# A tile's product within its chunk, issued one step sooner on TensorE

## The chip, the cores and the metric

The kernel runs on one core of a Trainium2 chip. The metric is the device time of one execution in microseconds (us). A time given for a kernel is the median over several executions.

## The reference

Three stages follow each other. The first is a recurrent attention (mLSTM) over 4 batches, 8 heads, 768 tokens and a head size of 40; the other two are dense layers over the 3072 tokens x 320 that it gives.

```python
for t in range(S):                                   # S = 768, for each batch and head
    m_new = np.maximum(f_gate[t] + m, i_gate[t])
    f_stab, i_stab = np.exp(f_gate[t] + m - m_new), np.exp(i_gate[t] - m_new)
    m = m_new
    C = f_stab * C + i_stab * outer(v[t], k[t])      # 40 x 40
    n = f_stab * n + i_stab * k[t]
    y[t] = sigmoid(o_gate[t]) * (C @ q[t]) / np.maximum(abs(n @ q[t]), 1.0)
x = relu(x @ w_in) ** 2 @ w_out                      # 3072x320, 320x2048, 2048x320
x = elu(x @ w_in2) @ w_out2
```

## The kernel before, in words

**Tiles.** The recurrence is computed by chunks of 128 tokens. A tile g is one chunk of one batch with its 8 heads, so there are 24 tiles: g = 4 * chunk + batch. Three tiles make a block, 8 blocks for each dense layer. A layer works through a block in 16 steps, one for each slice of 128 of the 2048 hidden columns. A step t (0 to 255, 0 to 127 for the first layer) issues on TensorE `first_product(t)`, 8 matmuls of 128x384 at L933 in float32r, and `second_product(t - 3)`, 9 matmuls of 128x320 at L947.

**What is between the two products.** The attention of tiles 3 to 23 is woven into the steps of the first layer. For tile g, `start_of(g)` is its first step s (1, 6 and 11 for tiles 3, 4 and 5; after that 16 * (g // 3 - 1) + 5 * (g % 3) - 1), and `tile_at(t, delay)` gives the tile whose s + delay is t. TensorE executes in the order in which it is written out by hand:

- step s: `scores(g)`, q times k for each head, L823, into the PSUM banks A0 and A1; it waits until tile g - 1 is finished (`den_ready`) and for the low part of q (`q_lo`)
- step s + 2: `state_added(g)`, 16 instructions at L838 (the chunk's own k and weighted v, into A2; for tile 3 it is in its step 3, and the last chunk has none), then `from_state(g)`, 6 instructions at L849 (q times the state of the chunks before, into A0; none for tile 3, which is of the first chunk)
- step s + 3: `within(g)`, 16 instructions at L858 (the weighted scores in `wts` times v, into A1)
- step s + 5: `x1_transposed(g)`, three transposes of the finished tile (L863 and L864)

These attention products are plain float32, which is two instructions for each.

**The other engines for tile g.** VectorE in step s multiplies the scores into `wts` (`weigh`, L629, two halves; each raises `p_ready`). `from_state` waits for the first half, `within` for both. In step s + 3 VectorE runs in this order: `update_state` (L640, L643), `add_inter` (L651), the low part of this step's activations (`glo`, L773, which needs ScalarE's L546, L549 and L550 behind `first_product(s + 3)`), in the first block the low parts of a later slice's weights (L688, L690), then `finish(g)`: L660 (waits for `within(g)` by `intra_ps`) to L673 (`den_ready`) and the copy L676 (`x_ready`). ScalarE splits the next tile's k (L443) and q (L448); GpSimd makes the low part of q (`split_q_lo`, L342, two halves), the mask (L347) and the weighted v (L359). A DMA queue (SP) loads the next tile's q and k (L258) when the low part of the present q is made, then k, v and o (L266) and the row of maxima (L247).

**Waits that bear on the moved call.**

```python
def within(g):
    kvo_loaded(pe, g)
    pe.wait_ge(s["p_ready"], 2 * g + 2)
```

Of the kernel before, what the change touches and what calls it, by code (L numbers as in the profile page):

```python
# [50 lines left out]
def start_of(g):  # L51

    if g < 2 * T:
        return (1, 6, 11)[g - T]
    return NF * (g // T - 1) + 5 * (g % T) - 1


def tile_at(t, delay):

    for g in range(T, TILES):  # L60
        if start_of(g) + delay == t:
            return g
    return None


def transposed_at(t):

    return 2 * T - 1 if t == NF - 1 else tile_at(t, 5) if t != NF else None


def mlstm_two_dense_layers(nc, gates_ends, gates_inner, qk, q_trios, kvo, w_all, m_dram, out):
    with ExitStack() as ctx:
# [734 lines left out]
        def _(pe):  # L807
            def scores(g):
                if g < B:
                    pe.wait_ge(s[f"qk_in_{g}"], 16)  # L810
                    q_h, k_h = q_raw(g), k_raw(g)
                else:
                    pe.wait_ge(s["k_lo"], with_state(g) + 1)
                    q_h, k_h = q3, k3
                if g >= T:
                    pe.wait_ge(s["den_ready"], g)
                if g == T:
                    pe.wait_ge(s["decay_ready"], 1)
                for u, bank in enumerate(score_banks(g)):
                    if g >= B:  # L820
                        pe.wait_ge(s["q_lo"], 2 * with_state(g) + u + 1)
                    for h in range(HH):
                        last = nc.tensor.matmul(bank[:, h * P:(h + 1) * P], k_h[:, u * HH + h, :], q_h[:, u * HH + h, :],  # L823
                                                start=True, stop=True)
                    last.then_inc(s["s_ps"], 1)

            def state_added(g):
                if chunk_of(g) == CH - 1:
                    return
                pe.wait_ge(s["wv_ready"], g + 1)  # L830
                if g == 0:
                    pe.wait_ge(s["a_col_ready"], 2)
                elif g <= T:
                    pe.wait_ge(s["state_ready"], g)
                else:
                    pe.wait_ge(s["xt_ready"], g)
                for h in range(H):
                    last = nc.tensor.matmul(A2[0:D, h * E:(h + 1) * E], k_of(g)[:, h, :], wv[:, h, :], start=True, stop=True)  # L838
                last.then_inc(s["dc_ps"], 1)

            def from_state(g):
                if chunk_of(g) == 0:
                    return
                pe.wait_ge(s["state_in"], 48 * (with_state(g) + 1))
                pe.wait_ge(s["trio_in"], 16 * (with_state(g) + 1))
                pe.wait_ge(s["p_ready"], 2 * g + 1)
                for i in range(TRIOS):
                    n = min(3, H - 3 * i)
                    last = nc.tensor.matmul(A0[:, 3 * i * EV:(3 * i + n) * EV], q_of_three[0:n * D, i, :],  # L849
                                            state_diag[0:n * D, i, 0:n * EV], start=True, stop=True)  # L850
                last.then_inc(s["inter_ps"], 1)
# [4 lines that stand above are left out]
                bank = score_banks(g)[1]  # L856
                for h in range(H):
                    last = nc.tensor.matmul(bank[:, h * E:(h + 1) * E], wts[g % 3][:, h, :], v_of(g)[:, h, :], start=True, stop=True)  # L858
                last.then_inc(s["intra_ps"], 1)
# [6 lines left out]
            def x1_transposed(g):  # L866
                pe.wait_ge(s["x_ready"], g + 1)
                if g == 0:
                    pe.wait_ge(s["p_ready"], 1)
                elif g < T:  # L870
                    pe.wait_ge(s["xt_ready"], g)
                else:
                    pe.wait_ge(s["state_ready"], to_state(g + 1))
                transposed(x1[g % 2], x1[g % 2][:, 2 * P:3 * P], x_bank(g))

            def x2_transposed(i, w):
                pe.wait_ge(s["acc_free"], i + 1)
                pe.wait_ge(s["rest_ready"], i + 1)
                pe.wait_ge(s["xt_ready"], TILES + i - T + 1)
                if i < T:  # L880
                    pe.wait_ge(s["den_ready"], TILES)
                transposed(x2[:, i, :], x2_rest[i % 2][:].rearrange("p a n -> p (a n)"), (A0, A1, A2)[w])
# [40 lines left out]
            def first_product(t):  # L923
                block, j = divmod(t, NF)
                if j == 0:
                    pe.wait_ge(s["xt_ready"], T * (block + 1))
                if block % BLOCKS == 0:
                    win_lo_done(pe, NF * (block // BLOCKS) + j)
                wait(pe, "relu_ready" if block < BLOCKS else "g_ready", t - 1)
                hi, lo = xth[block % 2], xtl[block % 2]  # L930
                parts = [(0, hi, 0), (3, hi, 0), (0, lo, 0), (1, hi, 1), (4, hi, 1), (1, lo, 1), (2, hi, 2), (2, lo, 2)]
                for i, (w, x, kk) in enumerate(parts):
                    last = nc.tensor.matmul(hps[t % 2][:, 0:NT], win[:, j, w, :], x[:, kk, :], start=(i == 0),  # L933
                                            stop=(i == len(parts) - 1))
                last.then_inc(s["h_ps"], 1)

            def second_product(t):
                block, j = divmod(t, NF)
                pe.wait_ge(s["glo_ready"], t + 1)
                if block % BLOCKS == 0:  # L940
                    pe.wait_ge(s["wout_lo"], NF * (block // BLOCKS) + j + 1)
                for u in range(T):
                    if j == 0:
                        wait(pe, "acc_free", T * block + u - T + 1)
                    cols = slice(u * P, (u + 1) * P)
                    for i, (g, w) in enumerate(((ghi, 0), (ghi, 1), (glo, 0))):
                        last = nc.tensor.matmul(acc[u][:, 0:DM], g[t % GR][:, cols], wout[:, j, w, :],  # L947
                                                start=(j == 0 and i == 0), stop=(j == NF - 1 and i == 2))
                    if j == NF - 1:
                        last.then_inc(s["g_used"], 1)  # L950
                if j < NF - 1:
                    last.then_inc(s["g_used"], T)

            for block in range(2 * BLOCKS):
                for j in range(NF):
                    t = NF * block + j
                    if j == 0 and block > 0:
                        second_product(t - LAG)
                    first_product(t)
                    if t in FIRST_STATES:  # L960
                        state_added(FIRST_STATES[t])
                    g = transposed_at(t)
                    if g is not None and g >= 2 * T:
                        x1_transposed(g)
                    g = tile_at(t, 0)
                    if g is not None:
                        scores(g)
                    g = tile_at(t, 2)
                    if g is not None:
                        if g > T:  # L970
                            state_added(g)
                        from_state(g)
                    g = tile_at(t, 3)
                    if g is not None:
                        within(g)
                    if BLOCKS - 1 <= block < 2 * BLOCKS - 1 and j in X2_STEPS:
                        w = X2_STEPS.index(j)
                        x2_transposed(T * (block + 1 - BLOCKS) + w, w)
                    if t >= LAG and j > 0:
                        second_product(t - LAG)  # L980
                    g = transposed_at(t)
                    if g is not None and g < 2 * T:
                        x1_transposed(g)
# [47 lines left out]
```

## Time and profile before

| | |
|---|---|
| median of 3 runs | 843.82 us (843.19 to 845.56) |
| the profiled execution's own time | 845.63 us |
| its span, first to last instruction | 843.5 us |
| granted TensorE clock, mean over the span | 0.982 |
| steps with attention on TensorE | 46 to 440 us, roughly |

The profiled execution took 845.63 us, of which 843.5 are its span and 2.1 lie around it. It was 1.8 us above the median of the runs. Positions below are microseconds from the start of the span. A row of the order of time names start, duration, engine (PE is TensorE's matmul, PEld its weight load, DVE VectorE, ACT ScalarE, POOL GpSimd), line, operation and operands; several neighbours of one kind are one row with their count (x16), and the brackets give idle time before the row and what ended it.

### The profile page before, as it was taken

The numbers are of one execution on the slowest core, as the hardware profiler recorded it, in microseconds if no ns is written. First come the engines' busy times: TensorE is split into PE (matmuls) and PEld (weight loads), VectorE is DVE, ScalarE is ACT, GpSimd is POOL, SyncE is SP. The second block draws the span as 40 slices with busy tenths as digits, with TensorE's granted clock in tenths as the row PEclk, the third lists the DMA queues.
The fourth block names the chain that finished last, engine by engine and source line by source line (L and its number), as shares of the span: only waits on it lengthen the run. The fifth ranks groups of instructions, "written<-read, shape, count | busy, mean of one in ns | idle before, by whom it ended". The sixth has DMA issues, their size and how long they took to land.

```text
span 843.5 us, 14970 instructions
## 1 busy us (share of the span) xinstructions
PE 833.7 (99%) x5568; PEld 821.9 (97%) x5568; DVE 467.3 (55%) x823; ACT 492.0 (58%) x1088; POOL 263.9 (31%) x291
## 2 busy tenths in 40 slices
PE   8999999999999999999999999999999999999998
PEld 7899999999999999999999999999999999999998
DVE  4798776665665766656636644443434444444442
ACT  4698676776766767677658754444444444444443
POOL 2654221322222222211102353333433333333332
PEclk7599999999999999999999999999999999999999
DMA  8685444453643443445132300000000000000000
GB/s 240 244 236 142 128 117 108 108 138 86 162 138 95 121 118 108 108 107 152 38 103 70 103 1 2 24 1 24 1 24 1 24 1 24 1 24 1 1 24 24
DMA packets 28256, 66.93 MB, mean 79 GB/s; under 512 B 9400, under 2 KB 15384, under 8 KB 25624
## 3 DMA queue, kind: packets, MB, share of 16 engines
q1 hardware_dynamic: 27608, 64.54, 27.1%
q10 hardware_dynamic: 576, 1.44, 0.5%
q8 instruction: 44, 0.72, 0.4%
q14 instruction: 28, 0.23, 0.1%
HBM read 60.87 MB, written 4.03 MB: 77 GB/s over the span
## 4 chain that ended last, share of the span: by engine, by line
PE 96%; DMA 2%; DVE 1%; POOL 0%; issue 0%; ACT 0%; SPq 0%; DVEq 0%
PE hps L933 42%; PE acc L947 40%; PE att L858 5%; PE att L823 2%; PE att L849 2%; PE att L838 2%; PE att L863 1%; DMA raw<-in_qk 1%; PE att L864 1%; DVE gate L618 0%; PE acc L823 0%; DMA x<-in_gates_ends 0%; DMA m_rows<-x 0%; DVE x L673 0%; POOL wout L384 0%
## 5 line engine op out<-in xcount | busy, mean ns | idle before, releaser
L933 PE MATMUL hps<-xth,win 128*128 128x384 f32 x1280 | 350.7, 339 | 0.0
L947 PE MATMUL acc<-wout,ghi 128*128 128x320 f32 x1536 | 347.5, 313 | 0.0
L933 PE MATMUL hps<-xtl,win 128*128 128x384 f32 x768 | 260.0, 339 | 0.0
L947 PEld LDWEIGHTS acc<-wout,ghi 128*128 128x128 f32 x1536 | 257.8, 188 | 0.0
L947 PE MATMUL acc<-wout,glo 128*128 128x320 f32 x768 | 237.7, 309 | 0.0
L933 PEld LDWEIGHTS hps<-xth,win 128*128 128x128 f32 x1280 | 229.5, 188 | 0.3
L431 POOL TENSOR_TENSOR glo<-hact,ghi 128x384 fp32r<-128x384 f32 x128 | 130.1, 1016 | 217.2 <-ACT ghi L593 217.2
L773 DVE TENSOR_TENSOR glo<-hact,ghi 128x384 fp32r<-128x384 f32 x128 | 80.2, 627 | 144.7 <-ACT hact L550 143.2
L933 PEld LDWEIGHTS hps<-xtl,win 128*128 128x128 f32 x768 | 144.9, 189 | 0.0
L947 PEld LDWEIGHTS acc<-wout,glo 128*128 128x128 f32 x768 | 144.1, 188 | 0.0
L588 ACT ACTIVATE hact<-hact 128x384 f32<-128x384 f32 x128 | 67.2, 525 | 130.4 <-DVE hact L795 130.4
L546 ACT ACTIVATE hact<-hps 128x384 f32<-128x384 f32 x128 | 62.5, 488 | 118.2 <-PE hps L933 117.0
L795 DVE TENSOR_SCALAR hact<-hps 128x384 f32<-128x384 f32 x128 | 71.2, 556 | 104.6 <-PE hps L933 104.6
L798 DVE SCALAR_TENSOR_TENSOR hact<-hact,hps 128x384 f32<-128x384 f32 x128 | 71.0, 555 | 76.6 <-ACT hact L588 76.6
L593 ACT ACTIVATE ghi<-hact 128x384 fp32r<-128x384 f32 x128 | 67.3, 526 | 74.5 <-DVE hact L798 74.5
L347 POOL TENSOR_SCALAR_AFFINE_SELECT wts<-wts 128x1024 f32<-128x1024 f32 x24 | 26.2, 1092 | 189.6 <-ACT wts L469 189.6
L342 POOL TENSOR_TENSOR q<-raw,q 40x512 fp32r<-40x512 f32 x40 | 51.9, 1315 | 84.7 <-ACT q L448 84.6
L549 ACT ACTIVATE ghi<-hact 128x384 fp32r<-128x384 f32 x128 | 67.2, 525 | 4.1
L550 ACT ACTIVATE hact<-hact 128x384 f32<-128x384 f32 x128 | 65.0, 508 | 0.0
L469 ACT ACTIVATE wts<-wts,a_col 128x128 f32<-128x128 f32 x192 | 60.4, 387 | 5.5 <-DMA wts<-m_rows 5.5
L618 DVE RECIPROCAL gate<-gate 128x320 f32<-128x320 f32 x24 | 51.5, 2145 | 0.1
L858 PEld LDWEIGHTS att<-kvo,wts 128*128 128x128 f32 x336 | 42.0, 198 | 0.2 <-issue 0.2
(136 smaller groups left out, 664.5 us busy)
## 6 DMA issues: line engine op xcount, KB each, us to landing
raw<-in_qk SPq DMA_DIRECT2D x20, 960.0 KB, 7.2
wts<-m_rows SPq DMA_DIRECT2D x24, 512.0 KB, 8.7
kvo<-in_kvo SPq DMA_DIRECT2D x21, 484.0 KB, 7.9
x<-in_w_all SPq DMA_DIRECT2D x12, 352.0 KB, 7.0
wts<-in_w_all SPq DMA_DIRECT2D x12, 352.0 KB, 3.0
q_of_three<-in_q_trios SPq DMA_DIRECT2D x20, 180.0 KB, 2.6
out_x<-hsum SPq DMA_DIRECT2D x16, 160.0 KB, 1.9
x<-in_w_all ACTq DMA_DIRECT2D x4, 352.0 KB, 6.7
```

The source lines that it names most:

```text
L431: nc.gpsimd.tensor_tensor(glo[t % GR][:], gfull[t % 2], f32(ghi[t % GR][:]), ALU.subtract)\
L546: nc.scalar.activation(relu[t % 2], hps[t % 2][:, 0:NT], ACT.Relu).then_inc(s["relu_ready"], 1)
L549: nc.scalar.activation(ghi[t % GR][:], relu[t % 2], ACT.Square).then_inc(s["ghi_ready"], 1)
L550: nc.scalar.activation(gfull[t % 2], relu[t % 2], ACT.Square).then_inc(s["g_ready"], 1)
L588: nc.scalar.activation(relu[t % 2], relu[t % 2], ACT.Exp).then_inc(s["e_ready"], 1)
L593: nc.scalar.activation(ghi[t % GR][:], gfull[t % 2], ACT.Copy).then_inc(s["ghi_ready"], 1)
L773: nc.vector.tensor_tensor(glo[t % GR][:], gfull[t % 2], f32(ghi[t % GR][:]), ALU.subtract)\
L795: nc.vector.tensor_scalar(relu[t % 2], hps[t % 2][:, 0:NT], 0.0, None, ALU.min).then_inc(s["hneg_ready"], 1)
L798: nc.vector.scalar_tensor_tensor(out=gfull[t % 2], in0=relu[t % 2], scalar=-1.0, in1=hps[t % 2][:, 0:NT], op0=ALU.add, op1=ALU.max).then_i ...
L858: last = nc.tensor.matmul(bank[:, h * E:(h + 1) * E], wts[g % 3][:, h, :], v_of(g)[:, h, :], start=True, stop=True)
L933: last = nc.tensor.matmul(hps[t % 2][:, 0:NT], win[:, j, w, :], x[:, kk, :], start=(i == 0), stop=(i == len(parts) - 1))
L947: last = nc.tensor.matmul(acc[u][:, 0:DM], g[t % GR][:, cols], wout[:, j, w, :], start=(j == 0 and i == 0), stop=(j == NF - 1 and i == 2))
```

## The change

`within(g)` is no longer called in step s + 3 but in step s + 2, directly behind `from_state(g)` and ahead of that step's `second_product`. For tile 3 that is behind `state_added(3)` in step 3. Nothing is added or left out, and no other engine's order is changed.

```diff
@@ -970,8 +970,6 @@
                         if g > T:
                             state_added(g)
                         from_state(g)
-                    g = tile_at(t, 3)
-                    if g is not None:
                         within(g)
                     if BLOCKS - 1 <= block < 2 * BLOCKS - 1 and j in X2_STEPS:
                         w = X2_STEPS.index(j)
```

## Rows read from the trace of the kernel before

**Rows 1.** Busy time by stretch: us, then each engine's busy time and count, clock, DMA.

```profile
46.00:98.00 52.00, 50.43 (x371) 48.52 (x371) 45.70 (x75) 42.07 (x98) 21.63 (x20) 1.00 0.69 190
98.00:440.00 342.00, 342.00 (x2455) 337.25 (x2455) 210.94 (x355) 235.52 (x526) 71.45 (x64) 1.00 0.42 112
```

**Rows 2.** Waits of TensorE's weight loads, 48 to 100 us: total, times, longest.

```profile
PEld att L823 <- issue: 2.4, 3, 1.3
```

**Rows 3.** Order of time, TensorE's matmuls around tile 15.

```profile
273.80 0.90 PE L849 MATMUL att<-state_diag,q_of_three 120*128 120x126 f32 x6
...
274.87 0.31 PE L947 MATMUL acc<-wout,glo 128*128 128x320 f32 x1
...
277.13 0.34 PE L933 MATMUL hps<-xtl,win 128*128 128x384 f32 x1
...
279.38 0.31 PE L947 MATMUL acc<-wout,glo 128*128 128x320 f32 x1
...
281.64 0.33 PE L933 MATMUL hps<-xtl,win 128*128 128x384 f32 x1
...
282.10 0.31 PE L947 MATMUL acc<-wout,glo 128*128 128x320 f32 x1
```

**Rows 4.** Order of time in three narrow stretches, weight loads around tile 15.

```profile
273.55 0.20 PEld L838 LDWEIGHTS att<-wv,kvo 128*40 128x40 f32 x3
...
274.01 0.53 PEld L849 LDWEIGHTS att<-state_diag,q_of_three 120*128 120x128 f32 x4
274.46 0.30 PEld L947 LDWEIGHTS acc<-wout,ghi 128*128 128x128 f32 x2
...
278.53 0.53 PEld L858 LDWEIGHTS att<-kvo,wts 128*128 128x128 f32 x4
278.98 0.30 PEld L947 LDWEIGHTS acc<-wout,ghi 128*128 128x128 f32 x2
```

**Rows 5.** Order of time, VectorE and TensorE, tile 21.

```profile
382.72 1.28 DVE L629 TENSOR_TENSOR wts<-wts,att 128x512 f32<-128x512 f32 x2
...
386.89 0.79 PE L849 MATMUL att<-state_diag,q_of_three 120*128 120x126 f32 x6
```

**Rows 6.** Order of time, tile 3 (VectorE, TensorE, ScalarE).

```profile
46.87 1.29 DVE L629 TENSOR_TENSOR wts<-wts,att 128x512 f32<-128x512 f32 x2
...
46.97 0.81 PE L838 MATMUL att<-wv,x 128*40 128x41 f32 x16
...
50.54 1.87 PE L858 MATMUL att<-x,wts 128*128 128x41 f32 x16
...
52.48 0.47 ACT L546 ACTIVATE hact<-hps 128x384 f32<-128x384 f32 x1
...
54.41 0.56 DVE L773 TENSOR_TENSOR glo<-hact,ghi 128x384 fp32r<-128x384 f32 x1
...
58.36 0.49 DVE L673 TENSOR_TENSOR x<-att,rden 128x320 f32<-128x320 f32 x1
```

**Rows 7.** Order of time, tile 4, GpSimd.

```profile
73.49 3.22 POOL L342 TENSOR_TENSOR q<-raw,q 40x512 fp32r<-40x512 f32 x2
```

**Rows 8.** Order of time, tile 5, ScalarE and VectorE.

```profile
88.90 0.49 ACT L546 ACTIVATE hact<-hps 128x384 f32<-128x384 f32 x1 [1.75 <-PE hps L933]
...
89.85 0.51 ACT L550 ACTIVATE hact<-hact 128x384 f32<-128x384 f32 x1
...
91.27 0.54 DVE L773 TENSOR_TENSOR glo<-hact,ghi 128x384 fp32r<-128x384 f32 x1
...
93.17 0.49 DVE L673 TENSOR_TENSOR x<-att,rden 128x320 f32<-128x320 f32 x1
```

**Rows 9.** Order of time, tile 7, GpSimd, VectorE and TensorE.

```profile
125.91 2.53 POOL L342 TENSOR_TENSOR q<-raw,q 40x512 fp32r<-40x512 f32 x2 [4.84 <-ACT q L448]
...
127.35 1.14 DVE L676 COPY x<-x 128x64 f32<-128x64 f32 x1
...
130.47 0.38 PE L863 MATMUL att<-ident,x 128*128 128x128 f32 x2
```

## What the change will do to the time

> **What bounds the kernel now.** I read the busy times by stretch first. Behind 98 us TensorE is busy without a gap through all steps that carry attention; in the first block, 46 to 98 us, it is idle for 1.6 us, and there VectorE is busy 45.7 of 52 us [rows 1]. So TensorE sets the time, and VectorE is next to it in the first block alone. The view of waits says where those gaps are: three times the weight loads of `scores` (L823) wait, 2.4 us in all [rows 2]. Their places follow from the order of time. `scores(4)` begins when VectorE ends `finish(3)` at 58.36 + 0.49 = 58.85 us [rows 6], `scores(6)` when it ends `finish(5)` at 93.17 + 0.49 = 93.66 us [rows 8], `scores(5)` likewise at 77.6 us. The clock is at its full level, 2.4 GHz, in both stretches [rows 1]. A TensorE instruction that vanished, a gap that the move puts into TensorE, and a `finish` that comes later in the first block all go straight into the time. Everything else is covered.
>
> **What a group costs where it is now.** From the last L933 ahead of `within(15)` to the first `glo` matmul of L947 behind it is 279.38 - 277.13 = 2.25 us; in the step after, without attention, the same stretch is 282.10 - 281.64 = 0.46 us [rows 3]. So `within` costs 1.79 us. Its 16 instructions are paced by their weight loads: four take 278.98 - 278.53 = 0.45 us, 0.112 each, hence 16 x 0.112 = 1.79 us [rows 4].
>
> **What it costs behind `from_state`.** The loads of L849 go at the same pace, four in 274.46 - 274.01 = 0.45 us, and the load of another group follows the last at that pace, with no pause [rows 4]. The way out is the same too: from the first L947 load to the `glo` matmul is 274.87 - 274.46 = 0.41 us behind L849 and 279.38 - 278.98 = 0.40 us behind L858 [rows 3, 4]. So 16 loads put in between cost 16 x 0.112 = 1.79 us, what they cost where they were. One exit from float32 to float32r goes, which costs about 0.09 us (0.38 us from the first L947 matmul to the `glo` one against 0.28 us without attention ahead); but the group also had an entry behind L933 where its first load ran under a long matmul, and that cover goes with it. The term is 0.00 us for each of 20 tiles. The transition L849 to L858 is not in the trace, so I keep bounds. Below: the exit's 0.09 us is won and the lost cover costs nothing, -1.7 us over 20 tiles. Above: the nearest dear transition is from L838 to L849, where three loads at 0.04 each take until 273.80 - 273.55 = 0.25 us, 0.13 us of it a pause [rows 3, 4]; 20 x 0.13 = +2.6 us. I take 0, since L849 into L947 is the nearer row: equally wide weights on both sides, and no pause.
>
> The Trainium skill, TensorEngine Tiling (Array Packing), Key Properties, says that changing the tiling mode drains TensorE. Trace and rule agree at L838 to L849 (40 columns to 128) [rows 3, 4]; whether 80 rows to 128 is such a change no row shows. Were it one, it would be the upper bound above.
>
> **Does the moved call wait?** It needs both halves of `weigh` instead of one. The second ends least early in tile 21, at 382.72 + 1.28 = 384.00 us, 2.9 us before L849 begins [rows 5]; of tiles 4 to 23 none is nearer. Its v is part of the load that `state_added` and the gates have used already. Tile 3 is the exception: VectorE begins `weigh` at 46.87 us and ends it at 48.16 us, while TensorE is through with L838 at about 46.97 + 0.73 = 47.70 us [rows 6]. TensorE will stand for some 0.5 us, with `second_product(0)` and step 4 queued behind. What follows: `first_product(4)`, over at 50.7 us, just behind the start of L858 [rows 6], ends 0.5 + 1.79 = 2.3 us later, at 53.0. ScalarE took it up at 52.48 us anyway, now at about 53.05; VectorE's L773 at 54.41 us [rows 6] would begin some 0.15 us later, and so would `finish(3)`, for which `scores(4)` already waits 1.3 us [rows 2]. The 0.5 us stall is thus swallowed by that wait: **+0.15 us** for tile 3. Without the wait in `scores(4)` it would be +0.5.
>
> **The other engines see step s + 3 late.** `within` now stands ahead of `second_product` of s + 2, so `first_product(s + 3)` ends 1.79 us later, although TensorE as a whole is level again one product later. ScalarE's L546 follows it at once, and through L550 the L773 of VectorE that stands ahead of `finish(g)`.
>
> Tile 5 pays for it in full. ScalarE had waited 1.75 us for the product, so L546 would begin at 88.90 + 1.79 = 90.69 us and L550 end at 89.85 + 0.51 + 1.79 = 92.15; L773 begins just behind, at 92.18 instead of 91.27 us: `finish(5)` is 0.9 us late, and `scores(6)` waits for its L673 already [rows 2, 8]. No `intra_ps` wait gives it back, since VectorE was not waiting for one. **+0.9 us**.
>
> Tile 4: VectorE is late enough by itself that L773 moves by only 0.1 us. But the split of q moves by 1.79 us: GpSimd's pair of L342 would begin at about 75.3 instead of 73.49 us, and takes 2.6 to 3.2 us [rows 7], until 77.9 to 78.5 us. The second half of `scores(5)` needs it at 78.05 us, so it waits 0 to 0.45 us. On the other side the weights' low parts then escape the overlap with L342 (-0.3). I take **+0.1 us**.
>
> Tiles 6 to 23: TensorE stands nowhere from there on [rows 1], and a move of 1.79 us counts only where less than that is in hand. `scores` stands behind the transposes and needs L673 and the end of L342, in tile 7 at 127.3 and 128.44 us, over 2 us ahead of it [rows 9]. The transposes are closer. In tile 7 the copy L676 takes 1.14 us and ends at 128.49 us, with GpSimd's L342 (125.91 + 2.53 = 128.44), though it copies only 64 columns [rows 9]. Both move by 1.79 us: to 130.28 us. The transposes' weights load 0.17 us ahead of 130.47 us [rows 9], at 130.30. With the 0.07 us that a released load needs (58.85 to 58.92) this is 0.05 us late, partly under the last L933. It is so for the tiles of the first two places in a block, 12 in all (in the third, q is split a step later); 12 x 0.02 = **+0.25 us**.
>
> The Trainium skill, SBUF — State Buffer, SBUF: two separate sides, has GpSimd and some VectorE operations lock one pair of ports for a whole instruction. Rows 9 agree. Without such a lock the copy would be over before L342, and the 0.25 would be 0.
>
> Sum: 0.00 + 0.15 + 0.9 + 0.1 + 0.25 = +1.4 us. Against the profiled execution, 845.6 + 1.4 = 847.0 us; against the median, which lies 1.8 us lower, 843.8 + 1.4 = **845.2 us**, 0.17% more. A measurement of this kernel tells about 0.3% (2.5 us) from nothing, so my forecast is no change.
>
> **The rivals.**
> 1. The saved exit is real: TensorE wins 0.09 us in each of 20 tiles, 1.7 us, against 1.4 us lost: 843.5 us. For it speaks the 0.38 against 0.28 us; against it that the group is paced by loads. Chance 0.14.
> 2. The transition L849 to L858 pauses, as L838 to L849: +2.6 + 1.4 = 4.0 us, 847.8 us. It decides from 0.06 us for a tile on. Against it stands L849 to L947. Chance 0.08.
> 3. The transposes become late in the 12 tiles: if `x_ready` comes 0.15 to 0.3 us behind the point at which they are due (0.05 by my sum, and GpSimd's start is the uncertain part), 12 x 0.2 = 2.4 us comes in place of 0.25: 847.4 us. From 0.12 us for a tile on it is slower by over 0.3%. Chance 0.11.
> 4. Faster beyond doubt: the exit is won and the first block loses nothing, because its waits (2.4 us) shrink with the group gone from step s + 3: -1.7 - 1.5 = -3.2 us, 840.6 us. Against it, those waits are for `finish`, which waits for L773 and not for `within`. Chance 0.04.
>
> My own sum keeps 0.63, range 844.0 to 846.6 us.
>
> **How the numbers follow.** The predicted time is the sum's. Range 843.0 to 848.0 us: it holds the sum's case, most of rival 1 and about two thirds of rivals 2 and 3. Faster by over 0.3% (under 841.3): rival 4, 0.04. Slower (over 846.35): half of rivals 2 and 3 and a tenth of my own case, as the size in the first block is uncertain, 0.17. Within: 0.79.
>
> **What the changed profile would show.** L858's loads directly behind L849's at 0.112 us, with 1.79 us from one to the next group's load; a wait of 0.4 to 0.5 us before L858 in tile 3; a shorter wait at the first L823 of the three, a longer one (about 1.5 instead of 0.66 us) at the third; L676 still ending with L342 and the transposes without a wait over 0.1 us. The prediction is wrong if L858 pauses behind L849, if the transposes or `scores` wait behind 98 us, or if the granted clock leaves its upper level there.

## The result: slower by 0.57%, outside the range

The changed kernel takes 848.70 us (median of 6, 848.02 to 850.40) against 843.51 us for the one before (median of 6, 842.83 to 845.56): ratio 1.0057, interval 1.0040 to 1.0074. The prediction was 845.2 us, 843.0 to 848.0, and 0.79 for no change. In a second measurement of both kernels (below, 6 and 29 executions) the ratio was 1.0044, interval 1.0030 to 1.0058.

The profiled execution took 848.02 us with a span of 845.9, which is 2.4 us above the profiled one of before, and it took 0.7 us less than the median of its kernel, while that of before lay 2.1 us above its own (845.63 against 843.51). So one trace against the other shows only half of the difference of the medians. The rest had to be looked for in more traces.

**What came as predicted.** The product within the chunk stands directly behind `from_state`. In the order of time of the changed kernel, tile 15 (TensorE's matmuls):

```profile
275.08 0.90 PE L849 MATMUL att<-state_diag,q_of_three 120*128 120x126 f32 x6
...
277.94 0.31 PE L947 MATMUL acc<-wout,glo 128*128 128x320 f32 x1
```

From the first L849 to the first `glo` matmul are 2.86 us, against 274.87 - 273.80 = 1.07 us before [rows 3]: the group costs 1.79 us here, to the hundredth what it cost in its old place. The transition has no price. In tile 3 TensorE waits for the second half of `weigh`, as expected, though for 0.25 us in this trace (0.5 in E2's) where 0.4 to 0.5 was foreseen (order of time, 47 to 50 us):

```profile
48.26 1.95 PE L858 MATMUL att<-x,wts 128*128 128x41 f32 x16 [0.25 <-DVE wts L629]
```

**What waits now.** The view of waits of the changed kernel, weight loads, first 48 to 100 us, then 100 to 440 us (total, times, longest):

```profile
PEld att L823 <- issue: 1.9, 2, 1.6
...
PEld att L823 <- POOL q L342: 0.2, 1, 0.2
```

```profile
PEld att L838 <- issue: 3.5, 14, 0.3
PEld acc L947 <- issue: 2.8, 6, 0.5
```

The L838 row was there before as well and is no wait for data. The L947 row is new: six waits of 0.47 us of the weight load each, and in the one worked out below the matmul comes 0.35 us late. Busy times by stretch, to lay beside [rows 1], show TensorE no longer without a gap behind 98 us:

```profile
46.00:98.00 52.00, 50.39 (x372) 48.60 (x370) 43.48 (x75) 42.08 (x98) 21.23 (x20) 1.00 0.65 179
98.00:440.00 342.00, 340.92 (x2442) 334.34 (x2442) 219.46 (x355) 233.48 (x524) 73.51 (x64) 1.00 0.42 114
```

One of the six, step s + 3 of tile 15, in the order of time of the changed kernel (ScalarE and the weight loads):

```profile
280.54 0.49 ACT L546 ACTIVATE hact<-hps 128x384 f32<-128x384 f32 x1 [2.56 <-PE hps L933]
...
281.91 1.04 ACT L448 ACTIVATE q<-raw 120x1024 fp32r<-120x1024 f32 x1
282.86 1.06 ACT L501 ACTIVATE x<-acc 128x320 f32<-128x320 f32 x3
...
283.38 0.30 PEld L947 LDWEIGHTS acc<-wout,ghi 128*128 128x128 f32 x2 [0.47 <-issue]
```

and the same work of ScalarE in the kernel before:

```profile
278.87 1.04 ACT L448 ACTIVATE q<-raw 120x1024 fp32r<-120x1024 f32 x1
279.82 1.22 ACT L501 ACTIVATE x<-acc 128x320 f32<-128x320 f32 x3
```

L501 empties the three accumulator banks at the end of a block. It stands in the block's step 2, which for the first tile of each block is just s + 3, and behind L448 in ScalarE's order. ScalarE waited 2.56 us for the late product, and everything behind it moved with it: L501 from 279.82 to 282.86 us, of which 1.28 us is that this trace is later as a whole by then (the first L849 of tile 15 at 275.08 against 273.80 us) and 1.76 us is the move. The next step's `second_product` starts a new accumulation in these banks, and was due one L933 behind 282.90, at 283.07 us; it began at 283.42 (PE), when the first copy was done. Six times 0.35 us are 2.1 us.

**Tile 5.** Order of time of the kernel before, weight loads:

```profile
93.73 0.97 PEld L823 LDWEIGHTS att<-q,k 120*128 120x128 f32 x8 [0.66 <-issue]
```

and of the changed kernel, VectorE and weight loads:

```profile
91.48 0.56 DVE L773 TENSOR_TENSOR glo<-hact,ghi 128x384 fp32r<-128x384 f32 x1 [1.46 <-ACT hact L550]
...
93.39 0.49 DVE L673 TENSOR_TENSOR x<-att,rden 128x320 f32<-128x320 f32 x1
...
93.95 0.97 PEld L823 LDWEIGHTS att<-q,k 120*128 120x128 f32 x8 [1.59 <-issue]
```

VectorE now waits 1.46 us for the product ahead of L773, and `scores(6)` waits 1.59 us instead of 0.66: 0.9 us more, as worked out. TensorE came to it 0.7 us sooner (93.95 - 1.59 = 92.36 against 93.73 - 0.66 = 93.07 us), thanks to tiles 3 and 4, so `scores(6)` starts only 0.2 us later, and the loss by the end of the first block is small in this trace.

Moving tiles 3 and 4 has a consequence that the prediction did not look for. ScalarE stands 2.67 us for the transfer of tile 6's q and k ahead of L443 (85.28 us), where it stood 0.50 us before. The same wait is 1.8 to 3.3 us in every trace below in which these two tiles are moved and 0.2 to 0.5 us in every one in which they are not. What it adds to the wait of `scores(6)` is not shown by itself: that wait is 1.59 us with tile 5 moved alone (E5) and 1.95 us with all three (E3).

### The profile page after: what moved, and what is told of

The parts are those of the page before. It is cut to its first block, busy times and chain, and to the rows that moved or that the text cites. A ratio compares the mean times of both kernels' runs of the same rounds, so it can differ in the third digit from the quotient of the medians.

```text
span 845.9 us, 14970 instructions
## 1 busy us (share of the span) xinstructions
PE 837.7 (99%) x5568; PEld 823.6 (97%) x5568; DVE 474.4 (56%) x823; ACT 490.4 (58%) x1088; POOL 265.6 (31%) x291
## 4 chain that ended last, share of the span: by engine, by line
PE 92%; DVE 2%; ACT 2%; DMA 2%; issue 1%; POOL 0%; ACTq 0%; SPq 0%; DVEq 0%
PE hps L933 41%; PE acc L947 39%; PE att L858 5%; PE att L823 2%; PE att L849 2%; PE att L838 1%; PE att L863 1%; DMA raw<-in_qk 1%; ACT q L448 1%; DVE gate L618 1%; PE att L864 1%; PE acc L823 0%; ACT hact L546 0%; POOL q L342 0%; DVE win L688 0%
## 5 line engine op out<-in xcount | busy, mean ns | idle before, releaser
L933 PE MATMUL hps<-xth,win 128*128 128x384 f32 x1280 | 350.7, 339 | 0.0
L947 PE MATMUL acc<-wout,ghi 128*128 128x320 f32 x1536 | 345.9, 312 | 1.1 <-ACT x L501 1.1
L947 PEld LDWEIGHTS acc<-wout,ghi 128*128 128x128 f32 x1536 | 258.6, 188 | 2.8 <-issue 2.8
L933 PE MATMUL hps<-xtl,win 128*128 128x384 f32 x768 | 259.8, 338 | 0.0
L947 PE MATMUL acc<-wout,glo 128*128 128x320 f32 x768 | 237.3, 309 | 0.0
L933 PEld LDWEIGHTS hps<-xth,win 128*128 128x128 f32 x1280 | 229.6, 189 | 0.3
L773 DVE TENSOR_TENSOR glo<-hact,ghi 128x384 fp32r<-128x384 f32 x128 | 84.9, 663 | 138.7 <-ACT hact L550 136.9
L933 PEld LDWEIGHTS hps<-xtl,win 128*128 128x128 f32 x768 | 145.0, 189 | 0.0
L947 PEld LDWEIGHTS acc<-wout,glo 128*128 128x128 f32 x768 | 144.0, 188 | 0.0
L546 ACT ACTIVATE hact<-hps 128x384 f32<-128x384 f32 x128 | 62.5, 488 | 119.4 <-PE hps L933 118.3
L342 POOL TENSOR_TENSOR q<-raw,q 40x512 fp32r<-40x512 f32 x40 | 52.8, 1337 | 105.6 <-ACT q L448 105.5
L858 PE MATMUL att<-kvo,wts 128*128 128x41 f32 x336 | 41.9, 287 | 0.0
```

Of the source, the lines that this page charges most:

```text
L546: nc.scalar.activation(relu[t % 2], hps[t % 2][:, 0:NT], ACT.Relu).then_inc(s["relu_ready"], 1)
L773: nc.vector.tensor_tensor(glo[t % GR][:], gfull[t % 2], f32(ghi[t % GR][:]), ALU.subtract)\
```

## The experiments

Fifteen kernels, in four groups, each timed in 5 rounds beside the kernel before. Two stretches were read from every trace as the starts of the first L933 of three steps: steps 0 to 17 (first block) and 17 to 255 (the late part). In some kernels added lines move the line numbers by 2 or 4: L825 or L827 is `scores`, L935 or L937 `first_product`.

| kernel | ratio to before | interval | steps 0 to 17, us | steps 17 to 255, us |
|---|---|---|---|---|
| before, first trace | | | 62.65 | 734.46 |
| changed, first trace | 1.0057 | 1.0040 to 1.0074 | 62.90 | 736.76 |
| E1 before again | 0.9998 | 0.9990 to 1.0007 | 62.29 | 734.46 |
| E2 changed again | 1.0044 | 1.0030 to 1.0058 | 64.76 | 736.68 |
| E3 tiles 3 to 5 moved | 1.0019 | 1.0010 to 1.0027 | 64.84 | 734.44 |
| E4 changed, q sooner from tile 6 | 1.0024 | 1.0015 to 1.0034 | 65.40 | 734.13 |
| E5 tile 5 moved | 1.0016 | 1.0004 to 1.0028 | 63.06 | 734.44 |
| E6 tiles 3 and 4 moved | 0.9990 | 0.9980 to 1.0000 | 62.29 | 734.44 |
| E7 as E4, finish first | 1.0006 | 0.9994 to 1.0018 | 62.75 | 734.09 |
| E8 as E7, q sooner from tile 4 | 1.0017 | 1.0003 to 1.0031 | 64.26 | 734.09 |
| E9 tiles 6, 9, ..., 21 moved | 1.0019 | 1.0009 to 1.0029 | 62.56 | 736.78 |
| E10 the other tiles from 7 on moved | 0.9997 | 0.9986 to 1.0008 | 62.50 | 734.36 |
| E11 before, q sooner from tile 6 | 0.9997 | 0.9987 to 1.0007 | 63.08 | 734.44 |
| E12 tiles 3 and 4 moved, q sooner from tile 6 | 1.0033 | 1.0019 to 1.0047 | 65.34 | 734.46 |
| E13 changed, q sooner from tile 7 | 1.0018 | 1.0006 to 1.0029 | 63.18 | 734.09 |
| E14 all but tile 5 moved, q sooner from tile 7 | 0.9999 | 0.9989 to 1.0008 | 61.68 | 734.09 |
| E15 as E13, finish first | 0.9991 | 0.9981 to 1.0002 | 62.37 | 734.09 |

The late part repeats to 0.1 us from trace to trace of the same kernel, the first block doesn't. The time ahead of the first L933, 34.3 to 36.9 us, is in neither stretch.

### E1 and E2: both kernels again

> The kernel before, unchanged, against itself: the ratio must be 1.000. The medians of before and after lie 5.2 us apart, the two traces 2.4 us. If the three waits of TensorE in the first block (2.4 us of weight-load waits between 48 and 100 us) differ from one execution to the next (theory 1), this trace has fewer of them, down to none, and a span near 841 us. If the 2.8 us that the traces don't show lie elsewhere (rival), this trace again has 2.4 us of waits there and a difference in another stretch.

> The changed kernel, unchanged, against the kernel before: ratio 1.004 to 1.007 as on record. Its trace should again show six waits of L947 of 0.35 us each for ScalarE's L501 behind 98 us (2.1 us), by both theories; the first block's waits are what may differ from the trace on hand (2.4 us).

E1: 844.72 us. Its waits at L823 add up to 2.0 us between 48 and 100 us: the first half of theory 1 falls, the waits of before don't vanish. E2: 849.09 us; the six waits are there again, and the late part is 736.68 us. But its first block takes 64.76 us, 1.86 us more than in the first trace of the same kernel. Busy times by stretch of E2 (the granted clock is the third number from the end):

```profile
93.00:96.00 3.00, 1.71 (x14) 1.75 (x15) 2.73 (x8) 2.23 (x7) 0.00 (x0) 1.00 0.88 206
96.00:100.00 4.00, 4.00 (x19) 3.96 (x19) 0.90 (x2) 0.49 (x1) 0.00 (x0) 0.57 0.98 274
```

and of the first trace of the changed kernel:

```profile
96.00:100.00 4.00, 4.00 (x27) 3.87 (x27) 0.59 (x2) 0.86 (x2) 0.00 (x0) 1.00 0.96 288
```

In E2 the clock was at its lower level, 1.2 GHz, for 3.4 of these 4 us (0.57 of full as the mean: 0.43 x 4 / 0.5 = 3.4), and 19 matmuls ran where 27 had. The wait of `scores(6)` ended 2.0 us before the fall began (weight loads, E2):

```profile
94.25 0.97 PEld L823 LDWEIGHTS att<-q,k 120*128 120x128 f32 x8 [1.98 <-issue]
```

This wait is 0.39 us longer than in the first trace, so about 1.5 us of the 1.86 are the fall's (an estimate from these two numbers).

The Trainium skill, TensorE: Matmul & The Clock Gate, HAM oscillation — how this bites in real kernels, tells of a TensorE that alternates between its two clocks when its work has gaps. The trace agrees in that the fall follows a gap; but the page's gaps are longer ones, and by its rule a wait of 2 us would bring no fall. Here the measurement decides: four traces have a fall behind waits of 1.95 to 2.56 us.

Such a fall takes 0.002 off the mean clock of an execution, and can be told from it where the mean holds nothing else. For that one must know that executions begin in two ways. In the first kind (the first trace of before is one; mean near 0.98) the profile records a short spell at the upper level, up to 8.96 us in that trace, then the lower level (0.50) up to 39.7 us. In the second kind (the first trace of the changed kernel; mean 1.000 but for falls) it records nothing until the clock is at its upper level near 40 us, and shows 1.00. That is a gap in the record and no full clock: at 37 to 40 us two L933 start 0.32 us apart in the first trace of the changed kernel as in that of before, and 0.18 us apart once the upper level is recorded. The executions of before of the second kind took 1.7 to 1.8 us more in the median in three of the four groups and 0.2 us more in the first.

Among the executions of the second kind, those of the changed kernel without a fall (mean 1.000) took 848.02 and 848.19 us, those with one (0.997 and 0.998) 849.75, 849.99 and 850.40 us. Those of before in E1 (1.000) took 844.69 to 845.77 us. So the changed kernel is about 2.8 us slower without the fall and 4.8 us with it.

### E3, E5 and E6: the first block, and its tiles

Against the kernel before:

```diff
                         from_state(g)
+                        if g < 2 * T:        # E3; g == 5 in E5; g < 5 in E6
+                            within(g)
                     g = tile_at(t, 3)
-                    if g is not None:
+                    if g is not None and not (g < 2 * T):
                         within(g)
```

> Only tiles 3 to 5 have their product within the chunk one step sooner, tiles 6 to 23 as before. If the part of the loss that the two traces don't show sits in the first block (theory 1), +2 to +3 us against before, ratio 1.0024 to 1.0036. If the first block costs what the two traces say (rival), +0.3 us, ratio 1.0004, and at the most the +1.15 us of the prediction.

> Only tile 5 has its product within the chunk one step sooner. Theory: VectorE's L773 comes 0.9 us later and with it finish(5), so the wait of scores(6) grows from 0.66 to about 1.5 us, and in executions in which the granted clock falls to its lower level for 3.4 us behind that wait another 1.7 us is lost: +0.9 us without the fall, +2.6 us with it, ratio 1.001 to 1.003. Rival (the clock falls for the attention work being in one piece or for no reason in the kernel): no fall here, +0.9 us.

> Only tiles 3 and 4 have their product within the chunk one step sooner. Theory: the waits ahead of scores(4) and scores(5) shrink or stay, TensorE comes to tile 5 up to 0.7 us sooner, and scores(6) waits for finish(5) as before: no change within 0.3 us, no fall of the clock unless the wait at scores(6) passes about 1.5 us. Rival (the loss of the first block is tile 3's own wait of 0.5 us and tile 4's): +0.5 to +1 us.

E3 took 846.37 against 845.03 us, between what its two theories gave, with the clock at its lower level for 3.4 us behind a wait of 1.95 us. E5 took 846.11 against 844.49 us: +1.6 us, where 0.9 was expected without a fall. Its trace has the wait at 1.59 us and no fall; of its 5 executions of the second kind one (848.15 us, mean 0.998) has the mark of a fall. E6 took 844.05 against 844.49 us, no loss, and its wait at `scores(6)` is 0.9 us. The 1.5 us of its expectation, above which a fall was to come, is shown by no run. The first block's loss is tile 5's; tile 3's own wait of half a microsecond (0.5 us in E6's trace) costs nothing.

### E9 and E10: the late part, by place in the block

Against the kernel before:

```diff
                         from_state(g)
+                        if g >= 2 * T and g % T == 0:      # != 0 in E10
+                            within(g)
                     g = tile_at(t, 3)
-                    if g is not None:
+                    if g is not None and not (g >= 2 * T and g % T == 0):
                         within(g)
```

> Only tiles 6, 9, 12, 15, 18 and 21, the first of a block each, have their product within the chunk one step sooner. Theory: this part alone makes ScalarE's copies of the accumulators (L501) late, since they stand in the step whose first product ends 1.79 us later, behind the split of q: six waits of L947 of 0.35 us, +2.1 us behind 98 us, nothing ahead of it, ratio 1.0025. Rival (the waits need all tiles moved, or are an effect of the group in one piece): under +0.5 us.

> Only the tiles from 6 on that are second or third of a block have it one step sooner. Theory: no wait of L947, some 0.1 us at the transposes of each of six second places, +0.1 to +0.6 us in all, ratio within 0.1% of 1. Rival (the group in one piece costs TensorE time by itself, 0.1 us for each tile): +1.2 us from 12 tiles, and as much again in the kernel with the first places.

Weight loads' waits from 100 to 440 us, first E9, then E10:

```profile
PEld att L838 <- issue: 3.2, 13, 0.3
PEld acc L947 <- issue: 2.8, 6, 0.5
```

```profile
PEld att L838 <- issue: 3.5, 14, 0.3
```

E9 has the whole loss of the late part with six tiles moved, 736.78 - 734.46 = 2.3 us; E10 with twelve moved has none, 734.36 us. E9 took 845.98 against 844.45 us, only 1.5 us more, but 2 of its 11 executions and 16 of the 35 of before are of the longer, second kind: within the first kind the medians lie 2.3 us apart, within the second 1.8 us. E10 took 844.09 us. The waits are shown to be those of the first places, and the transposes, of which I expected 0.25 us, cost nothing.

### E4, E11, E12 and E13: L448 out of the way of L501

```diff
                         if g is not None and g >= B:
                             split_k_hi(g)
+                        if g is not None and g >= 2 * T:      # g > 2 * T in E13
+                            split_q_hi(g)
                         g = tile_at(t, -2)
-                        if g is not None and g >= B:
+                        if g is not None and B <= g < 2 * T:      # g <= 2 * T in E13
                             split_q_hi(g)
```

> The changed kernel, but ScalarE splits q (L448) of tiles 6 to 23 one step sooner, directly behind k (L443), so that the copies of the accumulators (L501) are not queued behind it in the step in which the first product now ends late. Theory: the six waits of L947 (2.1 us) go, and with GpSimd's L342 out of the way of L676 the 0.1 us at the transposes of six tiles too: 2.5 us faster than the changed kernel, ratio to before 1.0027. Rival (the wait is for the product's lateness itself, not for L448 in between): the waits stay at 0.35 us each and the ratio at 1.0057.

> The kernel before, with q split one step sooner for tiles 6 to 23. Theory: nothing waits there in the kernel before, so no more than 0.4 us is to be won behind 98 us, ratio 0.9995 to 1; the 2.3 us that the same edit gave the changed kernel is then the repair of the copies' wait and no gain by itself. Rival: it gains as much here, ratio 0.997.

> The version that the runs so far point to: the product within the chunk one step sooner for tiles 3 and 4 alone (0.999 by itself), and q split one step sooner for tiles 6 to 23. Theory: the two small gains add up, 0.5 to 0.9 us below before, ratio 0.999. Rival (both are within what one measurement differs from the next): ratio 1.000.

E4 took 847.32 us, 1.8 us less than E2. The waits of L947 are gone and the late part is 734.13 us, 2.6 us less: the theory holds for the late part. Its first block is 0.6 us longer than E2's, so that 1.8 us of the 2.6 are left. E11 shows the edit to be worth nothing where nothing waits (734.44; 843.93 against 844.45 us). E12 was to be the better version and is the opposite, 847.42 against 844.45 us. The reason is in E4's order of time too (ScalarE):

```profile
84.07 1.06 ACT L443 ACTIVATE k<-raw 120x1024 fp32r<-120x1024 f32 x1 [2.99 <-DMA raw<-in_qk]
85.03 1.04 ACT L448 ACTIVATE q<-raw 120x1024 fp32r<-120x1024 f32 x1
85.98 0.47 ACT L546 ACTIVATE hact<-hps 128x384 f32<-128x384 f32 x1
```

Tile 6's q and k land late; ScalarE stands 3 us for them, and with q sooner does L448 ahead of L546. The wait of `scores(6)` grows to 2.6 us (2.4 in E12), and the clock falls behind it in both traces. In E12 7 of 12 executions took more than 847 us. E11 has the same order without harm: with tile 4 in its old place ScalarE stands only 0.3 us for that transfer. So tile 6 was left out:

> The changed kernel with q split one step sooner for tiles 7 to 23 (in the earlier run also for tile 6, whose q and k land late: there ScalarE stood 3 us for the transfer and then did L448 ahead of L546). Theory: five of six waits of L947 go at once, the sixth (tile 6 to 7) too, the late part is that of before, and at scores(6) the wait is 1.5 to 1.9 us instead of 2.4: 1 us faster than with tile 6, ratio to before 1.001 to 1.0018. Rival (tile 6 makes no difference): 1.0024 again.

Order of time of E13, ScalarE in tile 15's step s + 3, L448 no longer ahead of the copies:

```profile
279.72 0.51 ACT L550 ACTIVATE hact<-hact 128x384 f32<-128x384 f32 x1
280.13 1.07 ACT L501 ACTIVATE x<-acc 128x320 f32<-128x320 f32 x3
```

845.77 against 844.73 us, ratio 1.0018. The wait at `scores(6)` is 1.8 us, without a fall in this trace, but 3 of its 4 executions of the second kind have the mark of one. What is left is tile 5.

### E14: both causes out, 20 of 21 tiles moved

The edits of E5's kind (`g != 5`) and of E13 together.

> All tiles but tile 5 have their product within the chunk one step sooner, and q is split one step sooner for tiles 7 to 23. Both causes found are gone from it. Theory: the time of before or a little less, ratio 0.999 to 1.000, no fall of the clock behind 50 us in most executions. Rival (the move has another cost in it, such as the group in one piece): ratio above 1.0015.

844.30 against 844.73 us, ratio 0.9999. Weight loads' waits, 44 to 100 us:

```profile
PEld att L840 <- issue: 1.0, 4, 0.2
PEld att L825 <- issue: 0.6, 2, 0.3
PEld att L860 <- issue: 0.5, 1, 0.5
PEld att L825 <- POOL q L342: 0.2, 1, 0.2
```

`scores` hardly waits, and both stretches are the shortest or as short as any of the table. None of its 11 executions took over 845 us, and none of the 6 of the second kind has the mark of a fall. With both causes taken out the move costs nothing.

### E7, E8 and E15: finish ahead of L773

```diff
                             add_inter(g)
+                            if g < 2 * T:
+                                finish(g)
                         dve.wait_ge(s["g_ready"], t + 1)
...
-                        if g is not None:
+                        if g is not None and not (g < 2 * T):
                             finish(g)
```

> The changed kernel with q split one step sooner for tiles 6 to 23, and with VectorE's finish(g) of tiles 3 to 5 ahead of L773 instead of behind it, which is possible only because the product within the chunk is there a step sooner. Theory: finish(5) ends near 91.9 instead of 93.9 us, finish(3) and finish(4) 2 us sooner too, so that scores waits little in the first block, the clock doesn't fall, and the time is 1 to 2 us below before: ratio 0.998. Rival (the low part of q, GpSimd's L342, takes over as what scores waits for): the waits shrink by less than 1 us and the time is that of before.

> As the kernel of the run before it, and q of tiles 4 and 5 is split one step sooner as well. By the theory that L342 is what scores waits for next in the first block, another 0.3 to 1 us faster; by its rival (VectorE is full in the first block whatever the order) no difference between the two.

> All tiles moved, q sooner for tiles 7 to 23, and VectorE's finish(g) of tiles 3 to 5 ahead of L773. Theory: the earlier run of this kind lost at tile 6 what it won at tile 5 by its q; without that the waits of the first block are under 1.5 us in all and the time 0.5 to 1.5 us below before, ratio 0.9985. Rival: the wait for L342 (0.5 us each at tiles 4 and 5) keeps it at 1.000.

E7: 844.29 against 844.49 us. The wait of `scores(6)` is 0.5 us or less in its trace, but L342 takes over (weight loads' waits, 48 to 100 us):

```profile
PEld att L827 <- POOL q L342: 1.2, 2, 0.7
PEld att L827 <- issue: 0.5, 1, 0.5
```

E8, with q of tiles 4 and 5 sooner, loses again (845.71): `scores(6)` waits 2.3 us, and ScalarE waits 3.1 us (1.8 in E7) for k and q of tile 6 and then does L448 ahead of L546, as in E4; this trace has no fall of the clock. E15, the same repair without tile 6's q, took 844.35 against 844.73 us, 0.9991 with an interval that reaches over 1. None of the versions is faster than before beyond its uncertainty, though E15 and E14 are clearly better than the changed kernel.

## Why the prediction was wrong, point by point

- **The step that failed** is the one that closes tiles 6 to 23: "a move of 1.79 us counts only where less than that is in hand". The rule is right, and I applied it to `scores` and to the transposes, but not to what stands behind L448 on ScalarE in the same step. The copies of the accumulators (L501) do, once a block. They had less than 1.79 us in hand. The term should have been +2.1 us (6 x 0.35) for 0.00; the late part measured +2.3 us, and E9, E10 and E4 show it to be this and nothing else of any size.
- **Tile 5**: the mechanism was right, and 0.9 us is what the wait grew by in the first trace. The term was too small: in a good part of the executions the wait is longer (1.98 us in E2) and the granted clock falls to 1.2 GHz for 3.4 us behind it, which together cost a further 1.9 us (E2 against the first trace). I had named a fall of the clock as something that would make the prediction wrong, behind 98 us alone, and given it no case and no price. E5 measured +1.6 us for tile 5 alone. The first trace says +0.3 us for the whole first block, because moving tiles 3 and 4 brings TensorE 0.7 us ahead, which had no term either.
- **L849 to L858**: right, 1.79 us and no pause; rivals 1 and 2 are out. Behind 98 us, E13 to E15 against before leave -0.37 us for 18 moved tiles, 0.02 us each, where rival 1 wanted 0.09.
- **Tile 3 and tile 4**: TensorE stood in tile 3 as foreseen and it was swallowed; the sum of the two is -0.4 us or nothing (E6), against +0.25 predicted.
- **The transposes**: +0.25 predicted, none measured (E10). Rival 3 is out.
- **Rival 4** asked whether the first block's waits could shrink. They were 2.4 and 2.0 us in the two traces of before (all waits of `scores`, 48 to 100 us). They shrank where tile 5 stayed where it was, to 1.4 us in E6 and 0.8 us in E14, and with `finish` ahead of L773, to 1.7 us in E7 and 1.2 us in E15; the change as it stands left 2.1 to 2.5 us.

The sum as it should have been: +2.3 (late part), +0.3 to +0.9 (first block), and +1.9 in the executions with a fall: 2.6 to 5.1 us. The two measurements gave 4.1 and 5.2 us of median difference; the second is just above the sum, and how the ways of beginning are mixed in six executions can move such a median.

Does the long wait bring the fall? Waits of 1.95 us and more have a fall behind them in four traces (E2, E3, E4, E12), one of 2.34 us has none (E8), and none follows those of 1.84 us (E13) and 1.59 us (the first trace, E5). The executions of the second kind, in which a mean of 0.998 or less tells of a fall, say more. In the kernels whose traces have a wait of 1.59 us or more at `scores(6)` (the changed one, E3 to E5, E8, E12, E13), 14 of 29 have the mark. In the others, the kernel before among them, 1 of 79 has it, an execution of E7. So the falls come with the kernels that make `scores(6)` wait long, from 1 of 6 such executions in E8 to 4 of 4 in E12. What decides it within one kernel stays open.

## What to carry to other kernels

When a group is moved up in one engine's order, list every instruction of the other engines that stands behind the product that thereby comes late, through the whole step and in each kind of step (first, middle, last of a block), and compare the slack of each with the move; TensorE being level again one product later says nothing about them. A repair that starts work sooner on a queue in strict order must be looked at in the step in which its input lands last. And where a wait grows toward 2 us on a saturated TensorE, carry a fall of its clock as a case with its own price.

## What the hardware showed unexpectedly

One fall of the granted clock to 1.2 GHz in the middle of a busy stretch lasted 3.4 us in each of the four traces that have one and cost about 1.5 us by the estimate above. It began with TensorE busy again and not in the wait: 2.0 us behind its end in E2, 0.9 us in E4, 0.6 us in E3 and 0.3 us in E12. A granted clock of 1.00 at the start of a trace can be missing record: only the pace of the matmuls (0.32 us from one L933 to the next, against 0.18 us) shows it. And the move from L849, with 80 rows in its last instructions, to L858, with 128, took no pause at all, while the one from 40 columns to 128 (L838 to L849) takes 0.13 us before and about as much after.
